# First block of a one-core convolution and two-MLP kernel: all taps of the last 64 channels on TensorE, three tiles slice by slice, zeros while x is loading, and the last sums in halves

## The chip, the cores and the metric

The kernel runs on one core of one Trainium2 chip. The metric is the device time in microseconds of one execution; the time of a kernel is the median of its runs. The engines are called PE (TensorE), DVE (VectorE), ACT (ScalarE), POOL (GpSimd) and SP (SyncE, which here only issues DMAs). "L452" is line 452 of the kernel.

## What is computed

```python
def _attn_ref(x, weight):                 # x (4, 4096, 192), weight (8, 7)
    w = weight - np.max(weight, axis=-1, keepdims=True)
    w = np.exp(w)
    w = w / (np.sum(w, axis=-1, keepdims=True) + 1e-09)
    x_pad = np.concatenate([np.zeros((B, K - 1, D)), x], axis=1)
    idx = np.arange(S)[:, None] + np.arange(K)[None, :]
    x_unf = x_pad[:, idx, :].reshape(B, S, K, H, D // H)
    return np.einsum('hk,bskhg->bshg', w, x_unf).reshape(B, S, D)

def _moe_ref(x, w_gate, w_val, w_out):    # (16384, 192) -> 1536 -> 192
    gate = 1.0 / (1.0 + np.exp(-(x @ w_gate)))
    return gate * (x @ w_val) @ w_out

def _moe2_ref(x, w_in, w_out):            # 192 -> 2048 -> 192
    r = np.maximum(x @ w_in, 0.0)
    return (r * r) @ w_out

# reference: _moe2_ref(_moe_ref(_attn_ref(x, weight)))
```

A causal convolution of seven taps, whose weights are the softmax over a row for each of eight heads of 24 channels, is followed by a gated MLP and by a squared-relu MLP. All is in fp32.

## The kernel before

**Tiling.** The 4096 positions are cut into 32 blocks of 128. A block holds 128 positions of all four sequences, so each matmul streams 512 columns. Activations lie with channels on the partitions. Each fp32 factor is split into a rounded high part and a low part, and a product takes three fast matmuls: high by high, low by high, high by low. The 192 channels are three slices of 64. Slices 0 and 1 ("main") are 128 channels. Slice 2 is called "rest". Two matmuls on 64 rows each, one on the lower and one on the upper half of the partitions, run side by side: L452 and L453 make the gate and the value tile of the first MLP, L499 and L500 (main outputs) and L507 and L508 (rest outputs) sum the outward product in `acc`. I call such two matmuls a pair. A tile of the first MLP takes 9 pairs inward and 5 pairs outward.

**Order of the work.** PE's program is written out by hand. `gated(0)` is the first MLP of block 0: 12 tiles t. After the inward matmuls of tile t come the outward ones of tile t - 3. Tile t may overwrite its PSUM banks when DVE has taken tile t - 2 out of them (`prod_done`). ACT takes the sigmoid of a tile (L693), DVE multiplies it with the value (L851), ACT rounds it (`hi`), DVE subtracts (`lo`, L865). Then `gated(1)`, and a loop over the other blocks in which the second MLP of one block alternates with the first MLP of a later one.

**The first block.** SP loads x of block 0 (rest, then main), then the first weight pieces into four staging buffers. PE makes the softmax weights into per-channel columns `taps` (L621), transposes x (L565 rest, L569 main), and ACT copies the transposed x into `xT` (L705). DVE runs all seven taps of rest (L905, 256 columns each) and four taps of main (L914, L905, 512 columns); PE runs three taps of main as fp32 matmuls with diagonal matrices (L578), which DVE adds (L921). ACT rounds (`x0_hi`), DVE subtracts (L878 main, L882 rest; `x0_lo`). SP then spreads the rest rows to both halves (L309, four DMAs) and swaps the main halves (L300, L301). PE takes the first two tiles slice by slice: slice 0, then slice 2 when spread, then slice 1 when swapped (`first_tiles`).

**The weights.** Weights arrive in pieces; ACT rounds a piece (`piece_hi`, L645), DVE subtracts (`piece_lo`, L839; `first_lo`, L872, for parts of the first three pieces). A piece n from 4 on goes into the buffer of piece n - 4; SP issues piece 4 when all six parts of pieces 0 to 2 have been split (`w1_lo` at 6). In `gated(0)`, `FIRST_AT` sets where pieces 4 to 8 are split: piece 4 stands in ACT's and in DVE's queue ahead of tile 1, piece 5 ahead of tile 2, piece 6 ahead of tile 3. DVE's queue at tile t of `gated(0)` holds, in this order, two taps of the convolution of block 1, the piece, the product of tile t, the subtraction of tile t - 1.

**The end.** After the last sums, ACT copies half of them from PSUM, DVE adds, PE transposes, ACT and DVE copy, and SP stores rest (L334) and then main (L337).

## Time and profile before

| | |
|---|---|
| median of 3 runs | 2346.86 us (2346.43 to 2347.02) |
| the profiled execution's own time | 2346.62 us |
| its span in the trace | 2344.9 us |
| busy share of PE, DVE, ACT, POOL | 99%, 80%, 54%, 6% |
| granted TensorE clock, mean | 1.0 |
| first pair of the stream (L452) starts | 15.75 us |
| last store is issued | 2342.19 us |

The times in the rows below are microseconds from the start of the span, and the span is one execution on the one core. The profiled execution's own time is 1.7 us more than its span, and 0.24 us below the median of the runs. A row of a timeline gives start, duration, engine, line, operation, output and inputs, count, and in brackets how long the engine was idle before it and what released it.

### The profile page before, as it was taken

How to read it: one execution, taken by the hardware profiler on the slowest of the kernel's cores; microseconds unless marked ns; L12 is line 12 of the kernel's file. 1: busy time of each engine (PE TensorE's matmuls, PEld its weight loads, DVE VectorE, ACT ScalarE, POOL GpSimd, SP SyncE). 2: the span in 40 equal slices, each digit the busy share in tenths (PEclk: the TensorE clock that was granted, in tenths of full speed). 3: DMA queues.
4: the chain of work that ended last, by engine and by line, in shares of the span. 5: the costliest groups of instructions: out<-in, count | busy, mean ns of one | idle time of the engine just before them, and what ended most of it. 6: DMA issues, size and time to landing. Idle time of an engine off the chain costs nothing.

```text
span 2344.9 us, 54295 instructions
## 1 busy us (share of the span) xinstructions
PE 2331.7 (99%) x20518; PEld 1923.5 (82%) x20518; DVE 1884.5 (80%) x3969; ACT 1276.0 (54%) x2344; POOL 149.6 (6%) x121
## 2 busy tenths in 40 slices
PE   8999999999999999999999999999999999999999
PEld 6888888888888888888888888888888888888887
DVE  7778778788788787887878878788787787887856
ACT  5545555455554455545555545555555554455556
POOL 2200000000000000000000000000000000000000
PEclk9999999999999999999999999999999999999999
DMA  6111111111110111101111111111111111111101
GB/s 170 42 28 46 30 47 42 31 47 29 49 47 25 47 29 49 47 25 47 36 42 47 33 41 40 36 47 42 31 47 29 47 47 26 47 29 49 41 19 37
DMA packets 93695, 99.28 MB, mean 42 GB/s; under 512 B 8736, under 2 KB 77856, under 8 KB 93664
## 3 DMA queue, kind: packets, MB, share of 16 engines
q1 hardware_dynamic: 93408, 98.27, 16.9%
q10 hardware_dynamic: 256, 0.59, 0.1%
q8 instruction: 20, 0.33, 0.1%
q14 instruction: 11, 0.09, 0.0%
HBM read 19.27 MB, written 12.58 MB: 14 GB/s over the span
## 4 chain that ended last, share of the span: by engine, by line
PE 99%; DVE 0%; DMA 0%; ACT 0%; issue 0%; ACTq 0%; SPq 0%
PE hp L452 55%; PE acc L499 26%; PE acc L507 17%; PE hp L453 1%; PE acc L500 0%; PE acc L508 0%; PE hp L578 0%; DMA xs<-xs 0%; ACT L802 0%; PE hp L621 0%; PE acc L569 0%; DVE xs L878 0%; DVE hid_t L851 0%; DVE z L958 0%; DVE y L921 0%
## 5 line engine op out<-in xcount | busy, mean ns | idle before, releaser
L452 PE MATMUL hp<-xs,w 64*128 64x512 f32 x5760 | 1397.8, 386 | 3.3 <-DVE xs L878 1.5
L453 PE MATMUL hp<-xs,w 64*128 64x512 f32 x5760 | 1397.8, 386 | 0.0
L452 PEld LDWEIGHTS hp<-xs,w 64*128 64x128 f32 x5760 | 1059.6, 184 | 231.0 <-DVE xs L878 1.7
L453 PEld LDWEIGHTS hp<-xs,w 64*128 64x128 f32 x5760 | 1059.6, 184 | 0.0
L865 DVE TENSOR_TENSOR lo<-hid_t,hi 128x512 fp32r<-128x512 f32 x896 | 613.1, 687 | 63.7 <-ACT hi L663 59.5
L693 ACT ACTIVATE act_t<-hp 128x512 f32<-128x512 f32 x384 | 230.1, 599 | 694.9 <-PE hp L452 694.9
L499 PE MATMUL acc<-hi,wo 64*128 64x512 f32 x1792 | 549.0, 386 | 0.0
L500 PE MATMUL acc<-hi,wo 64*128 64x512 f32 x1792 | 549.0, 386 | 0.0
L696 ACT ACTIVATE act_t<-hp 128x512 f32<-128x512 f32 x512 | 302.7, 598 | 186.2 <-PE hp L453 186.2
L851 DVE TENSOR_TENSOR hid_t<-hp,act_t 128x512 f32<-128x512 f32 x384 | 264.9, 690 | 157.3 <-ACT act_t L693 148.9
L499 PEld LDWEIGHTS acc<-hi,wo 64*128 64x128 f32 x1792 | 329.7, 184 | 70.5
L663 ACT CAST hi<-hid_t 128x512 fp32r<-128x512 f32 x512 | 309.7, 611 | 73.2 <-DVE hid_t L855 73.2
L507 PE MATMUL acc<-lo,wo 64*128 64x512 f32 x896 | 345.9, 386 | 0.0
L499 PE MATMUL acc<-lo,wo 64*128 64x512 f32 x896 | 345.9, 386 | 0.0
L508 PE MATMUL acc<-lo,wo 64*128 64x512 f32 x896 | 345.9, 386 | 0.0
L500 PE MATMUL acc<-lo,wo 64*128 64x512 f32 x896 | 345.9, 386 | 0.0
L507 PE MATMUL acc<-hi,wo 64*128 64x512 f32 x896 | 345.9, 386 | 0.0
L508 PE MATMUL acc<-hi,wo 64*128 64x512 f32 x896 | 345.9, 386 | 0.0
L500 PEld LDWEIGHTS acc<-hi,wo 64*128 64x128 f32 x1792 | 329.7, 184 | 0.0
L855 DVE TENSOR_TENSOR hid_t<-act_t 128x512 f32<-128x512 f32 x256 | 176.2, 688 | 144.9 <-ACT act_t L696 142.9
L895 DVE STREAM_TRANSPOSE xT<-xin 32x128 f32<-32x128 f32 x960 | 258.6, 269 | 29.1
L905 DVE SCALAR_TENSOR_TENSOR y<-xT,taps,y 128x256 f32<-128x256 f32 (+1 forms) x381 | 247.7, 688 | 0.3
(83 smaller groups left out, 2141.2 us busy)
## 6 DMA issues: line engine op xcount, KB each, us to landing
xs<-xs SPq DMA_DIRECT2D x160, 256.0 KB, 3.7
xs<-y_rest SPq DMA_DIRECT2D x128, 128.0 KB, 3.0
out_dram<-stage SPq DMA_DIRECT2D x31, 384.0 KB, 2.6
xin<-in_x_dram SPq DMA_DIRECT2D x30, 384.0 KB, 3.4
moved<-y_parts SPq DMA_DIRECT2D x32, 128.0 KB, 2.2
moved<-z_parts SPq DMA_DIRECT2D x31, 128.0 KB, 2.2
stage<-in_moe_w_out_dram SPq DMA_DIRECT2D x7, 384.0 KB, 4.5
stage<-in_moe_w_in_dram SPq DMA_DIRECT2D x12, 128.0 KB, 3.0
```

What stands on the lines that cost most here:

```text
L452: low = pe.matmul(hp[:, 2 * pair, :], w[lower, wk, c], xs[lower, xk, :], start=s, stop=e)
L453: up = pe.matmul(hp[:, 2 * pair + 1, :], w[upper, wk, c], xs[upper, xk, :], start=s, stop=e)
L499: pe.matmul(acc[:, 0, :], w[lower], v[lower], start=s, stop=e)
L500: mm = pe.matmul(acc[:, 2, :], w[upper], v[upper], start=s, stop=e)
L507: pe.matmul(acc[:, 1, :], rest_w[lower], v[lower], start=s, stop=e)
L508: mm = pe.matmul(acc[:, 3, :], rest_w[upper], v[upper], start=s, stop=e)
L663: act.copy(hi[:, t % RING, :], hid_t[:, t % 4, :]).then_inc(hi2_done, 1)
L696: act.activation(act_t[:, t % 2, :], hp[:, 2 * (t // 2 % 2) + t % 2, :], ACT.Relu) \
L851: dve.tensor_tensor(hid_t[:, t % 4, :], hp[:, 2 * (t % 2) + 1, :], act_t[:, t % 2, :], ALU.mult).then_inc(prod_done, 1)
L865: dve.tensor_tensor(lo[:, t % RING, :], hid_t[:, t % 4, :], hi[:, t % RING, :].bitcast(F32), ALU.subtract).then_inc(done, 1)
L895: dve.transpose(dst, src).then_inc(xT_ready, 1)
L905: dve.scalar_tensor_tensor(out=y, in0=src, scalar=w, in1=y, op0=ALU.mult, op1=ALU.add) \
```

## The change

- SP loads x of block 1 into a buffer of its own (`acc_up`) right behind the first weights, instead of waiting until x of block 0 has been transposed. Each part of x has its own semaphore.
- DVE first writes 512 columns of zeros. PE multiplies them five times before it transposes the rest of x, and once behind it (`IDLE`). The two softmax matmuls (L621 before) now stand behind the rest transposes and ahead of the main ones.
- PE takes all seven taps of the rest channels (256 columns, fp32), DVE all seven of the main channels; the addition of the two (L921) is gone. ACT makes seven diagonals for the rest, in place of three for main. ACT and DVE round the rest sums straight from PSUM.
- Three tiles instead of two are taken slice by slice; tile 1 uses two banks of `acc`. The first weight pieces are cut at 384 columns instead of 256 for it. The swap of main is four DMAs of half the size: the high parts can go before the low parts are made. PE's wait for the low parts stands before the third pair of slice 1.
- In SP's queue x of block 2 is loaded behind the swap instead of ahead of it.
- At the end, the copies, additions, transposes and stores of the main channels go in two halves.

The core of the diff:

```diff
-    PE_TAPS = 3
+    FIRST_TILES = 3
+    IDLE = (5, 1)
...
-        pieces = [inward1(k, 0, CHUNK, (2 * P,)) for k in FIRST_SLICES] + [out_piece(w_out1, wo1, 0)]
+        pieces = [inward1(k, 0, CHUNK, (FIRST_TILES * P,)) for k in FIRST_SLICES] + [out_piece(w_out1, wo1, 0)]
...
+        def gate_of(j, t):
+            if isinstance(j, int) and j == 0 and t < 2:
+                return acc[:, 0:2, :] if t else hp[:, 2:4, :]
+            return hp[:, 2 * (t % 2):2 * (t % 2) + 2, :]
...
+            def swap_first():
+                xs = x0_home(0).bitcast(F32)
+                sp.wait_ge(x0_hi, 2)
+                sp.dma_start(xs[lower, 2, :], xs[upper, 0, :]).then_inc(high_swapped, 16)
+                sp.dma_start(xs[upper, 2, :], xs[lower, 0, :]).then_inc(high_swapped, 16)
+                sp.wait_ge(x0_lo, 2)
+                sp.dma_start(xs[lower, 3, :], xs[upper, 1, :]).then_inc(x0_swapped, 16)
+                sp.dma_start(xs[upper, 3, :], xs[lower, 1, :]).then_inc(x0_swapped, 16)
...
             load_x(0)
-            for n in range(FIRST):
+            for n in range(FIRST - 1):
                 load_piece(n)
             load_x(1)
+            load_piece(FIRST - 1)
             spread_x0(0)
+            swap_first()
             load_x(2)
-            swap_x0(0)
...
+                        if part == 2 and xk % 2:
+                            pe.wait_ge(x0_swapped, 32)
...
-                for k in range(PE_TAPS):
+                for k in range(K):
                     pe.wait_ge(tap_square, k + 1)
-                    mm = pe.matmul(hp[:, 2, :].rearrange("p (b s) -> p b s", b=B), diagonals[:, k, :], xT[:, 0:B, k:k + P],
-                                   start=k == 0, stop=k == PE_TAPS - 1)
+                    mm = pe.matmul(rest_conv, diagonals[:, k, :], xT[:, B:G, k:k + P], start=k == 0, stop=k == K - 1)
...
+            pe.wait_ge(zeroed, 1)
+            idle(IDLE[0])
             pe.wait_ge(heads, 8)
+            turn_rest(0)
+            idle(IDLE[1])
             pe.wait_ge(soft, 8)
...
-            turn_x(0)
+            turn_main(0)
             first_taps()
-            turn_x(1)
+            turn_rest(1)
+            turn_main(1)
...
+                elif prev is None and t == 3:
+                    pe.wait_ge(prod_done, 1)
...
             def first_conv():
-                dve.wait_ge(xT_copied, 1)
-                for k in range(K):
-                    tap(0, 1, k, k)
                 dve.wait_ge(xT_copied, 2)
...
+                dve.tensor_scalar(main, xT[:, 0:B, 0:P], taps[:, 0, 0:1], None, ALU.mult).then_inc(conv_step, K + 1)
+                for k in range(1, K):
+                    if k == K - 2:
+                        first_lo(0, 0)
+                    if k == K - 1:
+                        dve.wait_ge(x0_hi, 1)
+                        dve.tensor_tensor(y0_rest[:, 1, :, :], rest_conv, y0_rest[:, 0, :, :].bitcast(F32), ALU.subtract) \
+                           .then_inc(x0_lo, 1)
+                    tap(0, 0, k, K + k)
                 x0_low(0, 2)
+                first_lo(1, 0)
...
+                for half in range(2):
+                    b = slice(half * (B // 2), (half + 1) * (B // 2))
+                    sp.wait_ge(turn_copied, half + 2)
+                    sp.wait_ge(o_last, half + 2)
+                    sp.dma_start(to[:, b, 0:P], o_sb[:, b, 0:P]).then_inc(o_room, 16)
```

In DVE's program the convolution of block 0 stands right behind the copy of `taps`. Before (`y<-xT,taps` is a tap, `w<-stage,w` a part of a weight piece, `xs<-y,xs` the low part of main):

```order
L902 TENSOR_SCALAR y<-xT,taps 128x256 [waits xT_copied,soft]
L905 SCALAR_TENSOR_TENSOR y<-xT,taps,y 128x256 [waits conv_step] x6
L914 TENSOR_SCALAR y<-xT,taps 128x512 [waits xT_copied]
L882 TENSOR_TENSOR y_rest<-y,y_rest 128x256 [waits x0_hi]
L905 SCALAR_TENSOR_TENSOR y<-xT,taps,y 128x512 [waits conv_step] x3
L921 TENSOR_TENSOR y<-y,hp 128x512 [waits conv_step,conv_part]
L872 TENSOR_TENSOR w<-stage,w 128x256 [waits w_hi] x2
L878 TENSOR_TENSOR xs<-y,xs 128x512 [waits x0_hi]
```

The same place of the changed kernel:

```order
L992 TENSOR_SCALAR y<-xT,taps 128x512 [waits xT_copied,soft]
L986 SCALAR_TENSOR_TENSOR y<-xT,taps,y 128x512 [waits conv_step] x4
L953 TENSOR_TENSOR w<-stage,w 128x384 [waits w_hi]
L986 SCALAR_TENSOR_TENSOR y<-xT,taps,y 128x512 [waits conv_step]
L998 TENSOR_TENSOR y_rest<-hp,y_rest 128x256 [waits x0_hi]
L986 SCALAR_TENSOR_TENSOR y<-xT,taps,y 128x512 [waits conv_step]
L959 TENSOR_TENSOR xs<-y,xs 128x512 [waits x0_hi]
```

Seven taps of 256 columns and the addition are gone, three taps of 512 columns are new, and the low part of the rest now stands ahead of the last tap and reads PSUM.

In SP's queue, the DMAs behind the first weights, before (`xs<-y_rest` spreads the rest, `xs<-xs` swaps main, `xin` is x of block 2, the first `stage` load is piece 4):

```order
L309 DMA xs<-y_rest 64x4x128 [waits x0_lo]
L309 DMA xs<-y_rest 64x4x128 x3
L289 DMA xin<-in_x_dram 128x4x192 [waits x_turned]
L300 DMA xs<-xs 64x1024 [waits x0_lo]
L301 DMA xs<-xs 64x1024
L295 DMA stage<-in_moe_w_gate_dram 64x768 [waits w1_lo]
L295 DMA stage<-in_moe_w_val_dram 64x768
```

and in the changed kernel:

```order
L343 DMA xs<-y_rest 64x4x128 [waits x0_lo]
L343 DMA xs<-y_rest 64x4x128 x3
L331 DMA xs<-xs 64x512 [waits x0_hi]
L332 DMA xs<-xs 64x512
L334 DMA xs<-xs 64x512 [waits x0_lo]
L335 DMA xs<-xs 64x512
L313 DMA xin<-in_x_dram 128x4x192 [waits x_turned]
L319 DMA stage<-in_moe_w_gate_dram 64x768 [waits w1_lo]
L319 DMA stage<-in_moe_w_val_dram 64x768
```

The load of x of block 2 (384 KB) has moved from ahead of the swap to right ahead of piece 4, and the swap is four issues instead of two.

## Rows read from the trace of the kernel before

**Rows 1.** The page, busy time of each engine.
```profile
PE 2331.7 (99%) x20518; PEld 1923.5 (82%) x20518; DVE 1884.5 (80%) x3969; ACT 1276.0 (54%) x2344; POOL 149.6 (6%) x121
```

**Rows 2.** The page, costliest group: busy, mean ns, idle before it and its releaser.
```profile
L452 PE MATMUL hp<-xs,w 64*128 64x512 f32 x5760 | 1397.8, 386 | 3.3 <-DVE xs L878 1.5
```

**Rows 3.** Timeline of PE: first inward pair of tiles 4, 5 and 7.
```profile
27.68 0.39 PE L452 MATMUL hp<-xs,w 64*128 64x512 f32 x1
...
30.85 0.39 PE L452 MATMUL hp<-xs,w 64*128 64x512 f32 x1
...
37.20 0.39 PE L452 MATMUL hp<-xs,w 64*128 64x512 f32 x1
```

**Rows 4.** Timeline of DVE: piece 4, then products of tiles 2, 3, 5.
```profile
22.74 0.96 DVE L839 TENSOR_TENSOR w<-stage,w 128x768 fp32r<-128x768 f32 x1 [0.59 <-ACT w L645]
...
26.35 0.68 DVE L851 TENSOR_TENSOR hid_t<-hp,act_t 128x512 f32<-128x512 f32 x1
...
29.48 0.68 DVE L851 TENSOR_TENSOR hid_t<-hp,act_t 128x512 f32<-128x512 f32 x1
...
34.93 0.68 DVE L851 TENSOR_TENSOR hid_t<-hp,act_t 128x512 f32<-128x512 f32 x1
```

**Rows 5.** Windows: stretch, length, DVE busy (instructions), granted clock, DMA share, GB/s.
```profile
18.00:19.00 1.00, 0.86 (x2) 1.00 0.67 258
19.00:20.00 1.00, 0.00 (x0) 1.00 0.74 202
...
22.74:46.50 23.76, 23.58 (x40) 1.00 0.42 113
```

**Rows 6.** Timeline of ACT: piece 4.
```profile
21.88 0.83 ACT L645 CAST w<-stage 128x768 fp32r<-128x768 f32 x1 [0.45 <-DMA stage<-in_moe_w_val_dram]
```

**Rows 7.** Issues of piece 4's second half and of x (block 2), and times to landing.
```profile
18.49 0.60 SPq L295 DMA_DIRECT2D stage<-in_moe_w_val_dram  x1
...
stage<-in_moe_w_val_dram SPq DMA_DIRECT2D x1, 192.0 KB, 3.4
...
xin<-in_x_dram SPq DMA_DIRECT2D x1, 384.0 KB, 3.6
```

**Rows 8.** Timeline of DVE, first block: three main taps; four parts of pieces.
```profile
11.03 2.32 DVE L905 SCALAR_TENSOR_TENSOR y<-xT,taps,y 128x512 f32<-128x512 f32 x3
...
15.71 2.22 DVE L872 TENSOR_TENSOR w<-stage,w 128x256 fp32r<-128x256 f32 x4
```

**Rows 9.** The chain that ended last, first block: start, us.
```profile
13.63 0.69 DVE y L921
...
15.01 0.70 DVE xs L878
```

**Rows 10.** Timeline of ACT, first block: main copy; three diagonals.
```profile
7.11 0.58 ACT L705 COPY xT<-acc 128x512 f32<-128x512 f32 x1 [0.48 <-PE acc L569]
7.59 0.98 ACT L810 ACTIVATE hid_t<-ident,taps 128x128 f32<-128x128 f32 x3
```

**Rows 11.** Timeline of PE: main transposes of blocks 0 and 1; fp32 taps.
```profile
6.01 1.06 PE L569 MATMUL acc<-ident,xin 128*128 128x128 f32 x4
8.14 5.46 PE L578 MATMUL hp<-xT,hid_t 128*128 128x512 f32 x6 [1.07 <-ACT hid_t L810]
...
13.67 0.60 PE L569 MATMUL acc<-ident,xin 128*128 128x128 f32 x4
```

**Rows 12.** Timeline of SP: the four spreading DMAs.
```profile
11.14 2.67 SPq L309 DMA_DIRECT2D xs<-y_rest  x4
```

**Rows 13.** The end: the two last stores, and their times to landing.
```profile
2341.40 0.38 SPq L334 DMA_DIRECT2D out_dram<-stage  x1
2342.19 0.37 SPq L337 DMA_DIRECT2D out_dram<-stage  x1
...
out_dram<-stage SPq DMA_DIRECT2D x1, 256.0 KB, 2.3
out_dram<-stage SPq DMA_DIRECT2D x1, 128.0 KB, 2.0
```

More of the change, by code:

```diff
@@ L444, in _, with into @@
         def _(pe):
-            def into(pair, w, xs, c, order=(0, 1, 2), part=None):
+            def into(banks, w, xs, c, order=(0, 1, 2), part=None):
                 for n, k in enumerate(order):
@@ L451, in into @@
                         s, e = n == 0 and wk == xk, n == 2 and xk % 2 == 1
[L452 to L453 removed]
+                        if part == 2 and xk % 2:
+                            pe.wait_ge(x0_swapped, 32)
+                        low = pe.matmul(banks[:, 0, :], w[lower, wk, c], xs[lower, xk, :], start=s, stop=e)
+                        up = pe.matmul(banks[:, 1, :], w[upper, wk, c], xs[upper, xk, :], start=s, stop=e)
                 return low, up
@@ L460, in first_tiles @@
                     if part:
-                        pe.wait_ge(*((x0_swapped, 32) if FIRST_SLICES[part] == 1 else (x0_spread, 64)))
+                        pe.wait_ge(*((high_swapped, 32) if FIRST_SLICES[part] == 1 else (x0_spread, 64)))
                     pe.wait_ge(w1_lo, part + 1)
-                    for t in range(2):
-                        low, up = into(t, w1, x0_home(0), columns(t), FIRST_SLICES, part)
+                    for t in range(FIRST_TILES):
+                        low, up = into(gate_of(0, t), w1, x0_home(0), columns(t), FIRST_SLICES, part)
                         if part == 2:
@@ L645, in piece_hi, with first_hi @@
                     act.copy(h, staged(n, a, b)).then_inc(w_hi, 1)
+            def first_hi(n, part):
+                act.wait_ge(stage_loaded[n % STAGES], loaded[n])
+                a, b, h, _ = pieces[n][2][part]
+                act.copy(h, staged(n, a, b)).then_inc(w_hi, 1)
             def slot_free(kind, j, t, prev):
@@ L743, in z_copy @@
                     act.wait_ge(out2_done, T2 * NB)
-                    act.copy(acc_up[:, 0, :], acc[:, 2, :]).then_inc(z_copied, 1)
+                    for half in HALVES:
+                        act.copy(acc_up[:, 0, half], acc[:, 2, half]).then_inc(z_copied, 1)
                 else:
@@ L753, in turn_copy_last @@
                 act.copy(o_sb[:, :, P:D], turned_half(0)).then_inc(turn_copied, 1)
-                act.wait_ge(turned, 2)
-                act.copy(o_sb[:, :, 0:R], turned_half(2)).then_inc(turn_copied, 1)
+                for half in range(2):
+                    act.wait_ge(turned, half + 2)
+                    act.copy(o_sb[:, half * (B // 2):(half + 1) * (B // 2), 0:R], turned_main(half)[0]) \
+                       .then_inc(turn_copied, 1)
             def last_of(prev):
@@ L949, in z_add @@
             def z_add(j):
-                last = isinstance(j, int) and j == NB - 1
                 if not (isinstance(j, int) and j == 0):
                     dve.wait_ge(o_turned, O_SQUARES * j)
-                for n in (1, 0) if last else (0, 1):
-                    dve.wait_ge(z_copied, 2 * j + 1 + (1 - n if last else n))
+                for n in range(2):
+                    dve.wait_ge(z_copied, 2 * j + 1 + n)
                     if n:
@@ L1044, in squared @@
                         rest_lo(2, j, t - 1)
+            dve.memset(zeros.bitcast(F32), 0.0).then_inc(zeroed, 1)
             dve.memset(xT[:, :, 0:HALO], 0.0).then_inc(halo_ready, 1)
```

169 lines of the change are left out of this document (96 added, 73 removed).

## The prediction

> **What bounds the kernel now.** I read the page first. PE is busy for 99% of the span [rows 1], and its largest group was idle for 3.3 us in all, 1.5 of them ahead of the very first pair [rows 2]. Nothing between block 0 and the end waits, so the time is the start of PE's stream, plus its waits in block 0, plus the work, plus what follows the last sum. The change touches only the first and the last of these.
>
> Next I took PE's timeline of block 0. One tile of 14 pairs takes 3.17 us (30.85 less 27.68) [rows 3], so a pair takes 0.227. The stream starts at 15.75 and has 41 pairs ahead of tile 4, which are 9.3 us; without a wait tile 4 would start at 25.05. It starts at 27.68 [rows 3]: 2.6 us are lost in waits for the product of a tile and for swapped rows.
>
> Then DVE's timeline, for what PE waits on. Tile 4 needs the product of tile 2, which ends at 26.35 + 0.68 = 27.03 [rows 4], only 0.65 ahead of tile 4. Tile 5 needs that of tile 3, 30.16, which is 0.69 ahead of 30.85 [rows 3, 4]. For tile 7 the lead is 1.6 (35.61 against 37.20). And DVE is not resting: from 22.74 to 46.50 it is busy for 23.58 of 23.76 us [rows 5]. So in block 0 PE cannot run more than 0.65 ahead of now unless DVE's whole row of work moves ahead too. That row starts at 22.74 with the low part of piece 4, behind 0.59 of waiting for ACT [rows 4], which itself waited for piece 4 to land at 21.88 [rows 6]. **The reader is to see here that a load, not the convolution, holds what comes after tile 2.**
>
> **The change, part by part.** All sums go against the profiled execution, whose own time is 2346.62; the median of the runs is 0.24 more.
>
> *Start of the stream.* The main transposes no longer have two rest transposes ahead of them: four take 1.06 [rows 11], so two are about 0.5. ACT's copy of main moves from 7.11 to 6.6 and ends at 7.2 [rows 10]. DVE's seven main taps: three take 2.32 [rows 8], of which 0.7 is the last one's own length, so they follow each other every 0.8, each waiting for the one before. The first is a plain multiply, 0.5 (estimate). 7.2 + 0.5 + 6 x 0.8 = 12.5. A weight part of 384 columns and the low part of the rest stand between taps; four parts take 2.22 [rows 8], 0.55 each, and about half of each hides in the tap's own wait: 0.6 for the two. The convolution ends at 13.1, where now it ends at 13.63 + 0.69 = 14.32 [rows 9]. Rounding main, its low part and PE's start follow as now: L878 starts 0.69 behind the convolution and PE 0.74 behind that. PE starts at 14.5 instead of 15.75.
>
> This holds if the rest sums from PE are there in time. DVE's last tap is queued behind the rest's low part, which waits for ACT's rounding, which waits for PE's seventh tap. Six fp32 records of 512 columns take 5.46 [rows 11], about 0.87 each; 14 of 256 columns would be 6.0 at that pace. But that is the lower of the clock's two levels, 1.2 GHz: the four transposes at 6.01 take 1.06, the same four at 13.67 take 0.60 [rows 11], at 2.4 GHz. (The granted clock reads 1.00 throughout, so only the pace shows it.) ACT's diagonals, 0.33 each [rows 10], are ready by 9.1; at the upper level the last tap then ends near 10, far ahead of 11.5, where it begins to hold DVE. The trace shows PE's dense work from 8.14 becoming fast some 5 us later. [...] I take the upper level; at the lower one the price is 1.4 (below).
>
> *Three tiles by slices.* Slice 0: 9 pairs, 14.5 to 16.6. The rest's low part is made at about 12.3, four spreading DMAs take 2.67 to issue [rows 12] and 2.0 to land if they are like a 128 KB store [rows 13], so slice 2 starts at 16.6 to 16.9 and ends by 19.0. The four swaps are issued until 17.4 and land by 19.5, when PE comes to the first pair that needs low parts. Slice 1 ends at 21.1. Tile 3 needs the product of tile 0 (two steps of 0.6 and 0.7 behind its last pair at 19.5), runs from 21.3 and ends at 23.4. In the kernel before it ends at 27.68 - 5 x 0.227 = 26.55. **PE is 3.1 us ahead here.**
>
> *What is late next.* Outward tile 0 needs the product of tile 1, and ACT and DVE both have piece 4 queued ahead of that. When does piece 4 land? SP issues it when six parts of the first pieces are split: now 15.71 + 2.22 = 17.93 [rows 8]. In the changed kernel L878's successor starts at 13.8, but two parts stand ahead of the copy of the halo, ACT's two copies of block 1's x wait for that halo, and the last three parts wait for ACT behind these copies: 13.8 + 0.6 + 0.9 + 0.8 + 3 x 0.4 + 0.7 = 18.0, and the tolerance of such a sum is 0.3. So 0.1 later, in spite of the earlier convolution. And x of block 2, 384 KB, now goes out at about 17.4, right ahead of piece 4. Alone it took 3.6 to land [rows 7], against 2.0 for 128 KB [rows 13]. Its price for piece 4 lies between 0 (its bytes fit in the gaps: the DMA share is 0.67 and 0.74 from 18 to 20 [rows 5]) and 3.6 - 2.0 = 1.6. I take 0.6, since about half of it fits in these gaps and it has a start of 0.7. Piece 4 lands at 21.9 + 0.7 = 22.6, DVE's row of work starts 0.86 later [rows 4, 6] at 23.5, the product of tile 2 ends 4.3 later, at 27.8, and tile 4 starts then: 0.1 later than now, 0.2 with the slow first pair behind a wait (estimate). Of 3.1 us nothing is left. Bounds: -0.65 - 0.3 = -0.9 and 1.6 + 0.4 - 0.65 = +1.3.
>
> The Trainium skill, "DMA: Bandwidth & Descriptors", section "Queues, rings and completion order", says that each DMA engine consumes a queue's descriptors in ring order, so that a transfer issued ahead is served ahead. By it all of x would pass before piece 4; that is the second rival below.
>
> *The issues of piece 4 and of x* (SP) are hidden otherwise: x of block 2 is read in block 1 only. Zeros write a bank that is overwritten later, and their DVE memset, about 0.5, ends ahead of the first softmax step, which waits for its load. The earlier load of x of block 1 changes places with a weight piece of the same 384 KB, which is needed only near 18.
>
> *The end.* Now the stores go out at 2341.40 and 2342.19, the latter lands in 2.3, and 128 KB take 2.0 [rows 13]. Three stores cost three issues of 0.4: 2341.4, 2341.8, 2342.2. The halves of main are ready by then, since each step is shortened by a third or more. The last is 128 KB: 0.3 gained. Bounds 0 and 0.5.
>
> Sum: 2346.62 + 0.2 - 0.3 = 2346.5 for an execution like the profiled one, 2346.8 as a median.
>
> **The rivals.**
> (1) The clock stays at its lower level through PE's taps. For it: between the zeros and the taps stand only transposes and two tiny products. Then twelve records from 7.5 at 0.43 end at 12.7, rounding and low part move the last tap from 12.3 to 13.7, and all behind it, piece 4 too, by 1.4. Tile 4 starts 1.6 later than now: 2348.1, slower. It decides if the upper level comes later than about 10.
> (2) x of block 2 costs piece 4 its whole transfer, 1.6: tile 4 starts 1.1 to 1.2 later, 2347.8.
> (3) It costs nothing, and the parts are split as early as now: tile 4 at 27.0, 0.65 less and 0.3 at the end, 2345.9.
> (4) DVE's row of work does not bind, as when piece 4 can be taken up earlier or DVE catches up: the 3.1 stay, and 0.3: 2343.5. Against it: DVE has no gap from 22.74 on, and nothing of the change is taken out of that row.
>
> **How the numbers follow.** The likeliest case (2346.3 to 2347.3) has 0.47; rival (1) 0.15, (2) 0.16, (3) 0.15, (4) 0.07. The time is that of the first, 2346.8. The range 2345.4 to 2348.5 takes in (1) to (3) and leaves out (4) and some 0.08 of the rest. No change smaller than 0.2%, 4.7 us, can be told from none; even (4) stays within it. Faster 0.02, slower 0.01, no change 0.97.
>
> **What would show it.** PE's first pair at 14.5; end of tile 3 near 23.4; then a wait of more than 2 us for DVE ahead of the first outward pair and a second ahead of tile 4, which starts at 27.8; piece 4's rounding at 22.6; DVE without a gap behind it; the last store at 2342.1 less or plus what the head gives. Wrong if tile 4 starts before 27.0 or after 28.5, if PE's fp32 records of 256 columns go on at 0.43 behind 10, or if any wait turns up behind block 0.

## The result, and the profile after

| | before | changed |
|---|---|---|
| median, us | 2346.61 (22 runs) | 2349.64 (22 runs) |
| lowest to highest | 2346.43 to 2347.09 | 2347.90 to 2351.76 |
| profiled execution: own time, span | 2346.62, 2344.9 | 2349.22, 2347.5 |
| first pair, tile 4, tile 5, tile 7 start | 15.75, 27.68, 30.85, 37.20 | 13.96, 28.88, 33.70, 40.05 |

The ratio is 1.0014, 95% interval 1.0008 to 1.002. The changed kernel is 3.0 us slower. That is below the 0.2% that the prediction set as its bound, so its "no change" came true, but the time is outside its range of 2345.4 to 2348.5. It also scatters over 3.9 us, where the kernel before scatters over 0.7. Of the twelve runs of variant e17 below, two took 3452 and 9387 us and are left out of its row.

The page of the changed kernel first, busy time and costliest group (rows 1 and 2 of before answer to them):

```profile
PE 2335.6 (99%) x20532; PEld 2130.2 (91%) x20532; DVE 1886.8 (80%) x3967; ACT 1276.6 (54%) x2350; POOL 149.7 (6%) x121
...
L491 PE MATMUL hp<-xs,w 64*128 64x512 f32 x5751 | 1398.7, 387 | 2.6 <-DVE xs L959 2.0
```

This page hides the loss: PE is as busy as before, and its largest group waits less (2.6 us against 3.3 in [rows 2]). PE's waits from 13 to 60 us say more (who waited for whom, us, times, longest):

```profile
PE acc L540 <- DVE lo L946: 2.5, 1, 2.5
PE hp L491 <- DVE xs L959: 2.0, 1, 2.0
PE hp L491 <- DVE hid_t L932: 0.6, 1, 0.6
```

The first and the third, 3.1 us together, lie behind the first pair. That is about what the prediction expected. PE's timeline puts them in place: the taps on PE, the first pair, the last pair of tile 3 and the first outward pair, then tile 4:

```profile
6.28 3.57 PE L636 MATMUL hp<-xT,hid_t 128*128 128x256 f32 x14 [0.27 <-ACT hid_t L775]
...
13.96 0.49 PE L491 MATMUL hp<-xs,w 64*128 64x512 f32 x1 [1.96 <-DVE xs L959]
...
23.99 0.39 PE L491 MATMUL hp<-xs,w 64*128 64x512 f32 x1
...
26.85 0.46 PE L540 MATMUL acc<-hi,wo 64*128 64x512 f32 x1 [2.47 <-DVE lo L946]
...
28.88 0.79 PE L491 MATMUL hp<-xs,w 64*128 64x512 f32 x1 [0.61 <-DVE hid_t L932]
29.48 0.62 PE L491 MATMUL hp<-xs,w 64*128 64x512 f32 x1
29.90 0.62 PE L491 MATMUL hp<-xs,w 64*128 64x512 f32 x1
...
33.72 0.39 PE L491 MATMUL hp<-xs,w 64*128 64x512 f32 x1
...
40.06 0.39 PE L491 MATMUL hp<-xs,w 64*128 64x512 f32 x1
```

The head start is there. Tile 3's last pair starts at 23.99; in the kernel before tile 3 ended at 26.55. But tile 4 starts 1.2 us later than in [rows 3], and behind it pairs follow each other every 0.43 us instead of 0.227. From tile 4 to tile 5 it takes 33.70 - 28.88 = 4.82 us instead of 3.17. From tile 5 on the distance to the kernel before is a constant 2.85.

DVE and ACT, the rows that answer to [rows 4] and [rows 6], show why tile 4 is late (piece 4, then the products of tiles 2 and 3; piece 4 on ACT):

```profile
24.54 0.96 DVE L920 TENSOR_TENSOR w<-stage,w 128x768 fp32r<-128x768 f32 x1 [2.56 <-ACT w L707]
...
28.15 0.68 DVE L932 TENSOR_TENSOR hid_t<-hp,act_t 128x512 f32<-128x512 f32 x1
...
31.27 0.68 DVE L932 TENSOR_TENSOR hid_t<-hp,act_t 128x512 f32<-128x512 f32 x1
```

```profile
23.67 0.84 ACT L707 CAST w<-stage 128x768 fp32r<-128x768 f32 x1 [2.41 <-DMA stage<-in_moe_w_val_dram]
```

Both engines stand for 2.4 and 2.6 us before piece 4, with the products of tiles 1 and 2 queued behind it. SP's timeline, and how long x and the value half of piece 4 took to land, answer to [rows 7]:

```profile
17.21 0.59 SPq L313 DMA_DIRECT2D xin<-in_x_dram  x1
17.84 0.56 SPq L319 DMA_DIRECT2D stage<-in_moe_w_gate_dram  x1
18.45 0.60 SPq L319 DMA_DIRECT2D stage<-in_moe_w_val_dram  x1
...
xin<-in_x_dram SPq DMA_DIRECT2D x1, 384.0 KB, 4.3
...
stage<-in_moe_w_val_dram SPq DMA_DIRECT2D x1, 192.0 KB, 5.2
```

The value half is issued at the time of before (18.45, then 18.49) and takes 5.2 us instead of 3.4. That is the 1.8 by which piece 4 is late.

Windows of one microsecond show the second loss (length, PE busy, PEld, DVE, ACT, POOL, granted clock, DMA share, GB/s):

```profile
14.00:15.00 1.00, 1.00 (x10) 0.83 (x12) 0.93 (x3) 0.03 (x1) 0.00 (x0) 1.00 0.87 201
15.00:16.00 1.00, 1.00 (x8) 0.81 (x6) 0.00 (x0) 1.00 (x3) 0.00 (x0) 0.54 0.88 200
...
18.00:19.00 1.00, 1.00 (x10) 0.83 (x8) 0.70 (x2) 0.00 (x0) 0.00 (x0) 0.75 0.76 161
...
28.00:29.00 1.00, 0.39 (x6) 0.12 (x2) 1.00 (x3) 0.61 (x2) 0.00 (x0) 0.87 0.14 45
29.00:30.00 1.00, 1.00 (x6) 0.81 (x8) 1.00 (x2) 1.00 (x3) 0.00 (x0) 0.50 0.20 74
30.00:31.00 1.00, 1.00 (x8) 0.81 (x6) 1.00 (x3) 0.31 (x1) 0.00 (x0) 0.50 0.54 189
31.00:32.00 1.00, 1.00 (x6) 0.76 (x6) 1.00 (x3) 0.00 (x0) 0.00 (x0) 0.50 0.00 0
32.00:33.00 1.00, 1.00 (x10) 0.81 (x8) 1.00 (x2) 0.18 (x1) 0.00 (x0) 0.92 0.24 55
```

The granted clock is halved, 1.2 GHz, twice: from 15.1 to 18.5, behind the wait ahead of the first pair, and from 28.7 to 32.1, behind 3.1 us of waits. In a busy column both stretches look full; only the clock and the number of matmuls (6 to 8 instead of 10 to 12) show them. The first costs nothing here, since it only shortens the wait for piece 4. The second costs 1.65. Such stretches seem common in the changed kernel: the mean granted clock of this execution is 0.998, and 15 of the 22 runs have the same mean, the other seven 0.999.

**Ledger of the profiled execution:** tile 4 +1.2, the lower clock level behind it +1.65, the end about -0.25: +2.6 in the span. The end's rows answer to [rows 13]:

```profile
2344.16 0.38 SPq L368 DMA_DIRECT2D out_dram<-stage  x1
2344.65 0.97 SPq L373 DMA_DIRECT2D out_dram<-stage  x2
...
out_dram<-stage SPq DMA_DIRECT2D x3, 128.0 KB, 2.0
```

### The profile page after: what moved, and what is told of

Read it like the earlier page. It is cut to its first block, busy times and chain, and to the rows that moved or that the text cites. A ratio compares the mean times of both kernels' runs of the same rounds, so it can differ in the third digit from the quotient of the medians.

```text
span 2347.5 us, 54330 instructions
## 1 busy us (share of the span) xinstructions
PE 2335.6 (99%) x20532; PEld 2130.2 (91%) x20532; DVE 1886.8 (80%) x3967; ACT 1276.6 (54%) x2350; POOL 149.7 (6%) x121
## 4 chain that ended last, share of the span: by engine, by line
PE 99%; DVE 1%; DMA 0%; ACT 0%; issue 0%; DVEq 0%; SPq 0%; ACTq 0%
PE hp L492 50%; PE acc L541 23%; PE acc L549 16%; PE hp L491 6%; PE acc L540 3%; PE acc L548 2%; DMA stage<-in_moe_w_val_dram 0%; DVE y L986 0%; PE hp L611 0%; DVE w L953 0%; ACT xT L771 0%; DVE hid_t L932 0%; ACT w L707 0%; DVE y L983 0%; DVE w L920 0%
## 5 line engine op out<-in xcount | busy, mean ns | idle before, releaser
L986 DVE SCALAR_TENSOR_TENSOR y<-xT,taps,y 128x512 f32<-128x512 f32 x378 | 249.2, 697 | 0.1
```

The costliest lines, as they stand in the source:

```text
L986: dve.scalar_tensor_tensor(out=y, in0=src, scalar=w, in1=y, op0=ALU.mult, op1=ALU.add) \
```

## The experiments

Each ran beside the kernel before, whose median was 2346.86 beside e1, e3, e4 and e5, 2346.63 beside e2, e7, e8 and e9, 2346.78 beside e10, e12, e13 and e14, and 2346.64 beside e15, e16 and e17. These agree within 0.25. The changed kernel itself did not run again beside its variants, so they are compared with its 2349.64 of above. With 11 runs a kernel, the interval of a ratio is about 0.0009 to either side (2.1 us), so small differences are read from the timelines. Variants marked "before" are made from the kernel before, all others from the changed kernel. The starts and the span are those of the one profiled execution of each.

| kernel | median (lowest to highest) | first pair | tile 4 | tile 5 | tile 7 | span |
|---|---|---|---|---|---|---|
| e1 | 2346.78 (2345.92 to 2348.04) | 14.84 | 27.80 | 31.12 | 37.47 | 2345.1 |
| e5 (before) | 2347.91 (2347.59 to 2348.31) | 15.58 | 28.68 | 31.86 | 38.20 | 2345.9 |
| e7 | 2346.78 (2345.88 to 2348.59) | 15.19 | 28.29 | 33.05 | 39.40 | 2346.9 |
| e9 | 2346.51 (2345.42 to 2348.38) | 14.84 | 27.67 | 30.98 | 37.40 | 2344.9 |
| e3 | 2349.32 (2347.20 to 2351.92) | 15.00 | 30.10 | 33.41 | 39.81 | 2347.8 |
| e2 | 2349.93 (2348.59 to 2351.11) | 14.84 | 30.41 | 33.90 | 40.25 | 2347.7 |
| e10 | 2349.12 (2348.90 to 2349.68) | 15.35 | 30.79 | 34.12 | 40.51 | 2347.9 |
| e8 | 2348.19 (2346.21 to 2349.21) | 15.16 | 28.58 | 31.90 | 38.31 | 2347.5 |
| e4 (before) | 2346.48 (2346.27 to 2347.06) | 15.57 | 27.85 | 31.02 | 37.37 | 2344.8 |
| e14 | 2349.76 (2348.87 to 2350.54) | 13.96 | 25.90 | 32.02 | 40.07 | 2347.5 |
| e12 | 2347.84 (2346.53 to 2348.29) | 14.03 | 26.38 | 31.33 | 37.81 | 2345.2 |
| e13 (before) | 2348.28 (2347.85 to 2348.55) | 15.57 | 27.56 | 31.88 | 38.36 | 2346.0 |
| e15 | 2346.65 (2345.90 to 2347.51) | 14.83 | 27.09 | 30.40 | 36.80 | 2345.3 |
| e16 (before) | 2346.62 (2346.32 to 2347.32) | 15.58 | 27.41 | 30.59 | 36.93 | 2344.6 |
| e17 | 2346.05 (2345.07 to 2347.02) | 14.83 | 26.43 | 29.74 | 36.14 | 2345.3 |

### Where x of block 2 is loaded: e1, e5, e7

e1 takes the changed kernel and loads x of block 2 behind piece 6:

```diff
+            for n in range(FIRST, SECOND_HALF + 1):
+                load_piece(n)
             load_x(2)
-            for n in range(FIRST, PIECES1 + 6):
+            for n in range(SECOND_HALF + 1, PIECES1 + 6):
                 load_piece(n)
```

> The changed kernel with one move in SP's queue: x of block 2 is loaded behind pieces 4 to 6 instead of ahead of piece 4. Theory A (the load ahead of piece 4 holds DVE's row of work, and PE's wait for it then costs the clock): piece 4 is rounded at about 22.0 instead of 23.67, tile 4 starts near 27.2 instead of 28.88, the wait ahead of the first outward pair falls from 2.5 to under 1 us, no stretch at half clock behind it, and the time is about 3.2 us less than the changed kernel's 2349.6, so 2346.4. Theory B (the half clock comes from something else, the zeros or the early start): tile 4 starts 1.7 earlier, but the half-clock stretch behind it stays, 2348.0. Theory C (piece 4 is late for another reason, since its own issue is no earlier): no change, 2349.6.

It gives back the whole loss: 2346.78. The value half lands in 3.4 us again, and piece 4 is taken up at 22.58, 1.1 earlier, though this execution's first pair was 0.9 later:

```profile
22.58 0.83 ACT L709 CAST w<-stage 128x768 fp32r<-128x768 f32 x1 [1.62 <-DMA stage<-in_moe_w_val_dram]
```

e5 is the counterpart, the kernel before with its load of x of block 2 moved behind the swap and so right ahead of piece 4:

```diff
-            load_x(2)
             swap_x0(0)
+            load_x(2)
```

> The kernel before with x of block 2 loaded behind the swap instead of ahead of it, as the change does. Theory A (this move alone delays piece 4): piece 4 is rounded 1 to 1.8 us later than 21.88, tile 4 starts 0.4 to 1.2 later than 27.68, and if PE's wait gets long enough the clock falls too: 2347.0 to 2347.8 without the fall of the clock, up to 2349.4 with it. Rival (the delay comes from the four swaps or from the other traffic of the changed kernel): 2346.6.

This one move costs 1.05 us, and none of its runs is as fast as the slowest of the kernel before beside it (2347.34). Piece 4 is taken up at 22.90 instead of 21.88 [rows 6], and tile 4 starts at 28.68, 1.0 later. The clock does not fall in its profile, and the scatter stayed at 0.7.

```profile
22.90 0.83 ACT L645 CAST w<-stage 128x768 fp32r<-128x768 f32 x1 [1.33 <-DMA stage<-in_moe_w_val_dram]
```

e7 loads x of block 2 ahead of the spread instead:

```diff
             load_piece(FIRST - 1)
+            load_x(2)
             spread_x0(0)
             swap_first()
-            load_x(2)
```

> The changed kernel with x of block 2 loaded ahead of the spread of the rest (it is issued near 7 us, when its buffer is free) instead of behind the swap. Theory A (only its place ahead of piece 4 matters): piece 4 is rounded about 3.6 behind its issue as in the kernel before, near 22.2, tile 4 starts at 27.2 to 27.8, and the time is that of the version with the load behind piece 6, 2346.8 or a little less, 2346.3. Rival (any early place collides with the first weights and with x of block 1 and delays the taps): the first pair starts later than 14.8 and the time is 2347.5 or more.

The median is that of e1, 2346.78. Its profiled execution is one of the slowest, 2348.59, and has the lower clock level from 28.0 to 31.4 (tile 4 to tile 5 takes 4.76 us); the fastest runs, 2345.9, are 2.7 below it. So the order of the loads explains the median and not the scatter. The landing of the value half tells the two orders apart in eleven profiles: 5.2 to 5.6 us where x goes out right ahead of it (changed, e2, e3, e14, e15), 3.3 or 3.4 where it does not (before, e1, e7, e9, e12, e17).

### The clock: e3, e2, e10, e8

e3 puts ten matmuls into a bank that is overwritten later, into PE's wait ahead of the first outward pair:

```diff
                     pe.wait_ge(xT_copied, 4)
+                    for _ in range(10):
+                        pe.matmul(acc[:, 3, :], w1[:, 0, 0:P], w1[:, 0, 0:N], start=True, stop=True)
                     pe.wait_ge(prod_done, 2)
```

> The changed kernel with ten matmuls on weights that are already there, written to a bank that is overwritten later, in PE's wait ahead of the first outward pair of block 0 (the output is the same). Theory A (half clock because PE stood still for 2.5 us): the stretch at 0.50 granted clock from 28.9 to 32.1 is gone, tile 4 still starts at 28.9, and 1.5 us are saved: 2348.1, with less scatter. Rival (the clock falls whatever PE does there, or because of what lies before): no gain, 2349.6, or worse by up to 0.5 if the fill delays the outward pair.

The lower level behind the wait is gone in the profile (1.00 from 26 to 32), but the time is the same, 2349.32. This execution was slow in another place: PE's taps took 5.35 us instead of 3.57, and the chain behind them was later by 1.0 at the first pair (15.00) and by 1.2 at piece 4 (taken up at 24.89):

```profile
4.82 1.02 PE L684 MATMUL hp<-soft_w,act_t 8*128 8x7 f32 x4
5.77 1.11 PE L629 MATMUL acc<-ident,xin 128*128 128x128 f32 x4
6.69 5.35 PE L638 MATMUL hp<-xT,hid_t 128*128 128x256 f32 x14
```

These are the paces of the lower level (four main transposes 1.11, against 0.60 at 13.67 in [rows 11]), in spite of the zeros. So both of the prediction's cases happen with the same program up to that place. Among the ten profiles with zeros, PE has the faster pace by 4.8 in three (changed, e12, e14), and only near 11 in seven (e1, e3, e7, e8, e9, e15, e17). Why is not known. No run settles whether it changes from one execution to the next or goes with the chip: e12 and e14 ran on one chip, the seven late ones on three others, and the chip of the changed kernel is not on record. Note that e3's profile loses as much as that of the changed kernel (own times 2349.57 and 2349.22) with no stretch at the lower level behind tile 4: a late start ahead of the late piece 4 costs as much as an early start with the fall behind it.

e2 leaves out the zeros:

```diff
-    IDLE = (5, 1)
+    IDLE = (0, 0)
```

> The changed kernel without the six zero matmuls. Theory A (the zeros decide only when PE's clock first rises, and a fast start is paid back in the wait for piece 4): the softmax matmuls and the fp32 taps run at the slower pace in every run, the first pair starts at 15.0 instead of 13.96, piece 4 and tile 4 move with it by about 1.1, but PE is busier just before and the half-clock stretch behind tile 4 is gone or rarer: 2349.3 to 2350.0, and less scatter than 2347.9 to 2351.8. Rival B (the zeros themselves bring the later fall of the clock, and nothing else is lost): 2348.0. Rival C (the zeros give what they seem to give, 1 us or more of an earlier start): 2350.7 or more.

The median is 2349.93, not to be told from 2349.64. PE's taps take 5.45 us, and the clock falls before the end of the wait of 4.1 us ahead of the first outward pair. So theory A had the time right, but the stretch at the lower level is not gone. Where the clock rises early, the first pair starts at 13.96 instead of 14.84, 0.9 sooner; in seven of the ten profiles with zeros it does not rise early.

e10 is e2 with three fp32 matmuls in the wait ahead of the first outward pair:

```diff
                     pe.wait_ge(xT_copied, 4)
+                    for _ in range(3):
+                        pe.matmul(acc[:, 3, :], ident[:], w1[:, 0, 0:N].bitcast(F32), start=True, stop=True)
                     pe.wait_ge(prod_done, 2)
```

> The changed kernel with its six zero matmuls taken away and three fp32 matmuls on loaded data put ahead of the first outward pair instead, so that the program is as long as the changed one (ten more matmuls had brought one more load of program code at the very end; the output is the same). To be compared with the version without zeros, 2349.93. Theory A (half clock behind tile 4 comes from PE's wait for piece 4): no stretch at half clock from 28 us on in the profile, and 1 to 1.5 us less than 2349.93, so 2348.5 to 2349. Rival (the half clock has another cause): same as without zeros, 2349.9.

The windows of e2 and then of e10 (26 to 32 us, clock in the column ahead of the DMA share):

```profile
28.00:30.00 2.00, 1.86 (x9) 1.61 (x10) 2.00 (x4) 1.77 (x4) 0.00 (x0) 0.50 0.64 190
30.00:32.00 2.00, 2.00 (x16) 1.65 (x14) 2.00 (x5) 1.45 (x3) 0.00 (x0) 0.76 0.34 121
```

```profile
28.00:30.00 2.00, 1.25 (x10) 0.99 (x10) 2.00 (x5) 2.00 (x5) 0.00 (x0) 1.00 0.69 205
30.00:32.00 2.00, 1.40 (x12) 1.03 (x12) 2.00 (x5) 1.62 (x4) 0.00 (x0) 1.00 0.12 45
```

With the wait filled the level stays up, and the scatter falls from 2.5 to 0.8 us. The mean granted clock says the same of all runs: 0.998 or 0.999 in the eleven of e2, 1.000 in nine of e10's and 0.999 in two. This shows that the fall comes from PE standing idle, and that it makes most of the scatter of e2. The median falls by 0.8 only. In e2's profile the slow pairs are mostly the outward ones of tile 0, in a time in which tile 4 would have waited for DVE's product in any case: from the start of piece 4 on DVE, tile 5 is 8.06 us away in e2 and 7.67 in e10. And the 2349.12 of e10 are still 2.3 above the kernel before, without any fall: that part is the late start with piece 4 behind x.

Idleness does not make the clock fall every time (e1 has waits of 2.3, 1.7 and 0.6 us and 1.00 throughout), and the fall is not the only source of scatter. With the zeros in, the runs of the two other kernels with a filled wait still lie 4.7 (e3) and 3.0 us (e8, below) apart, although ten of e8's eleven have a mean clock of 1.000.

e8 is e7 with eight zeros ahead of the first pair and five fills ahead of the first outward pair:

```diff
+                    for _ in range(5):
+                        pe.matmul(acc[:, 3, :], w1[:, 0, 0:P], w1[:, 0, 0:N], start=True, stop=True)
...
             turn_main(1)
+            idle(8)
             gated(0, None)
```

> As e7_x2_early, with eight zero matmuls more ahead of the first pair and five matmuls on loaded weights ahead of the first outward pair (the output is the same). Theory A (what is left of the scatter is half clock after PE has stood still): no stretch at half clock in the first 40 us, and a time of 2346.0 with less scatter, 0.3 under e7_x2_early. Rival (once piece 4 is on time, the clock's falls are hidden in DVE's row, and the fills can only delay the first pair when the clock is low): same as e7_x2_early or up to 0.5 more.

Tile 5 starts at 31.90, 1.15 earlier than in e7, and yet the time is 2348.19, 1.4 more. The loss is at the other end: the last store has been issued at 2343.87, and the span ends 3.6 us later, where in the changed kernel it is 1.9 (2345.62 to 2347.5). The queue that loads instructions has one transfer more than in all other kernels, and it lies right behind that last store:

```profile
q8 instruction: 21, 0.34, 0.1%
```

The program is longer by thirteen matmuls. That the load is the cause is inferred from its place; no run isolates it. (The expectation of e10 puts such a load down to ten more matmuls. Those were e3's, and e3's profile has 20 transfers and the end of the others.)

### The end alone: e4

The kernel before with only the last sums halved.

```diff
...
-                sp.wait_ge(turn_copied, 2)
-                sp.wait_ge(o_last, 2)
-                sp.dma_start(to[:, :, 0:P], o_sb[:, :, 0:P]).then_inc(o_room, 16)
+                for half in range(2):
+                    b = slice(half * (B // 2), (half + 1) * (B // 2))
+                    sp.wait_ge(turn_copied, half + 2)
+                    sp.wait_ge(o_last, half + 2)
+                    sp.dma_start(to[:, b, 0:P], o_sb[:, b, 0:P]).then_inc(o_room, 16)
...
```

> The kernel before with the halved end alone. Theory A: the last store is 128 KB instead of 256 KB and is issued at the same time, 0.3 us less: 2346.3. Rival: the extra instructions and the third store cost as much as the smaller store gives, 2346.6.

The median is 0.38 below that of the kernel before, which the interval alone does not tell from nothing. The profile agrees: tile 7 starts at 37.37 (0.17 later than in [rows 3]) and the span is 0.1 shorter, so 0.3 are gained, as predicted.

### Splitting the first pieces sooner: e9

On top of e7, the last parts of the first pieces are split ahead of the copy of the halo (the last positions of block 0, which the convolution of block 1 needs), on both engines:

```diff
             first_hi(2, 0)
+            for n in range(3):
+                first_hi(n, 1)
             act.wait_ge(halo_ready, 2)
             for n in range(2):
                 xT_copy(1, n)
-            for n in range(3):
-                first_hi(n, 1)
...
             first_lo(2, 0)
-            keep_halo(0)
             for n in range(3):
                 first_lo(n, 1)
+            keep_halo(0)
```

> As e7_x2_early, and the last three parts of the first pieces are split ahead of the copy of the halo and of the copies of block 1's x on ACT and DVE, so that piece 4 can be issued sooner. Theory A (piece 4's landing sets DVE's row of work and so tile 4): the issue of piece 4 moves from 17.9 to 17.2, where SP's four swaps end, and the time falls by 0.5 to 0.7 against e7_x2_early, to about 2345.8, faster than the kernel before. Rival (something else in DVE's row binds, or block 1's x becomes late): no gain.

Piece 4 is on ACT at 22.04 with no wait. Seven runs lie at 2345.4 to 2346.6 and four at 2348.0 to 2348.4, with nothing between. Two cases of the clock would explain that, but it is not shown: the profile is of a run of the faster group, and the mean granted clock reads 0.999 in all four slow runs and in six of the seven fast ones. The median, 2346.51, tells only how many runs fell in which group.

### The pieces on another engine: e14, e12, e13

What remained was rival (4): is the head start worth its 3 us when piece 4 does not stand ahead of the products? e14 gives the low parts of pieces 4 to 6 to GpSimd and splits each a tile later:

```diff
-        FIRST_AT = {1: [4], 2: [5], 3: [6], 4: [7], 6: [8]}
+        FIRST_AT = {2: [4], 3: [5], 4: [6], 5: [7], 6: [8]}
...
+            for n in range(FIRST, SECOND_HALF + 1):
+                (a, b, h, l), = pieces[n][2]
+                pool.wait_ge(w1_lo, split_upto[n - 1])
+                pool.wait_ge(w_hi, split_upto[n])
+                nc.gpsimd.tensor_tensor(l, staged(n, a, b), h.bitcast(F32), ALU.subtract).then_inc(w1_lo, 1)
...
-                        piece_lo(n)
+                        if n > SECOND_HALF:
+                            dve.wait_ge(w1_lo, split_upto[SECOND_HALF])
+                            piece_lo(n)
```

> The changed kernel with the low parts of pieces 4 to 6 made by GpSimd instead of VectorE, and each of the pieces 4 to 7 rounded by ScalarE one tile later. Theory A (after tile 2 only DVE's row of work behind piece 4 holds PE): the wait of 2.5 us ahead of the first outward pair is gone, tile 4 starts near 25.8 although piece 4 lands as late as before, no half clock behind it, and the time is 2346.6 - 1.9 - 0.3 = 2344.4 or up to 1 us more where the clock rises late. Rival (PE is held by DMA or by the clock itself): more than 2347.

It missed by 5 us. Tile 4 did come to 25.90, three microseconds sooner than in the changed kernel, but tile 5 only at 32.02, behind a wait of 2.6 us for DVE's product. The clock was at its lower level from 32.1 to 35.6, so that tile 5 took 4.88 us instead of 3.17, although the expectation had no such stretch. DVE's and GpSimd's timelines show where the wait comes from:

```profile
27.08 4.29 DVE L991 SCALAR_TENSOR_TENSOR y<-xT,taps,y 128x512 f32<-128x512 f32 x2
...
32.48 1.14 DVE L991 SCALAR_TENSOR_TENSOR y<-xT,taps,y 128x512 f32<-128x512 f32 x2
```

```profile
24.78 6.30 POOL L469 TENSOR_TENSOR w<-stage,w 128x768 fp32r<-128x768 f32 x3 [21.37 <-ACT w L712]
```

The same two taps take 4.29 us beside GpSimd and 1.14 behind it; 4.29 is about the length of two of its instructions (2.1 each). The Trainium skill, "SBUF — State Buffer", section "SBUF: two separate sides", says that the two engines share a pair of ports under an exclusive lock, taken by a DVE instruction with two SBUF inputs against a GpSimd one that reads SBUF. By it each tap waits for a whole GpSimd instruction, and the rows agree.

e12 adds e14's edit to e9, and e13 adds it to the kernel before.

> As e14_after_pool, with x of block 2 loaded ahead of the spread and the last parts of the first pieces split ahead of the halo copy. Theory A: piece 4 is early, and nothing stands between the tiles: tile 4 starts near 25.4, time 2344.0, the fastest so far. Rival (with DVE's row gone, the start and the swaps bind and the earlier piece 4 gives nothing more): the same as e14_after_pool.

> The kernel before with the same move of three low parts to GpSimd. It tells what the change to the first block is worth once DVE's row does not bind. Theory A: the waits ahead of tile 4 in the kernel before (swapped rows, product of tile 0) stay, 25.05 + 2.3 = 27.4 for tile 4, only 0.3 less than now: 2346.3, so that the changed head is worth some 2 us over it. Rival (the kernel before gains as much, and the changed head gives nothing even then): 2344.5.

Both missed for the same reason: PE stands for 1.48 and 0.99 us ahead of tile 5, for DVE's product. e13 costs the kernel before 1.5 us.

### The same order without GpSimd: e15, e16, e17

These change only the line `FIRST_AT` above. The splits stay on ACT and DVE and stand one tile later: e15 on the changed kernel, e16 on the kernel before, e17 on e9.

> The changed kernel with the splits of pieces 4 to 7 (on ScalarE and on VectorE) one tile later in their order, and nothing on GpSimd. VectorE then takes product 1 and its low part in the 2.6 us in which it stood before piece 4 at 22 to 24.5, and the outward product of tile 0 can follow tile 3 at once. Theory (the head start of the new first block is real, 2.3 us, and was lost only because piece 4 stood ahead of product 1): tile 4 at 26.0 instead of 28.88, tile 5 at 29 to 30.5 instead of 33.70, no stretch at the lower clock level behind them, VectorE then sets the pace (0.95 for a piece + 0.6 + 0.6 + 0.95 for the taps, 3.1 a tile); 2345.5 in all, between 2344.3 and 2347. Rival (the head start is used up later whatever stands there: VectorE's whole row of pieces, products and taps until 45 us has no room): tile 4 at 26 but the tiles from 7 on at or behind their place, 2348 to 2349.6.

> The kernel before with the same one edit of the order, nothing on GpSimd. Its tile 3 ends at 26.55 and its tile 4 starts at 27.68, so only 1.1 of wait is there to be won at tile 4, less what VectorE's row binds at tiles 5 to 7 (0.1 to 0.2 each). Theory: tile 4 at 27.3 to 27.7, 2346.4 (2345.8 to 2346.9). It should lie 1 to 2.3 us above the changed kernel with the same edit if the head start is real; the rival has the two the same, or the changed one slower as it was without the edit.

> The same edit on the version with x of block 2 loaded ahead of the spread of x of block 0 and the last splits of the first pieces ahead of the copy of the halo. Piece 4 lands about 1.6 us sooner there, so less hangs on the order: theory 2345.0 (2343.8 to 2346.5), tile 4 at 25.8 to 26.2, the same as the changed kernel with the edit or up to 0.5 faster, and less scatter than the 3 us of the version without the edit if the stretch at the lower clock level comes from the wait at tile 4. Rival (the scatter comes from when the clock first rises): scatter of 2 to 3 us as before.

e15 takes off all of the loss: 2346.65, 3.0 less than the changed kernel, with x of block 2 where it was. DVE now works in the time in which it stood (the product of tile 1, a low part and two taps, then piece 4):

```profile
21.67 0.69 DVE L932 TENSOR_TENSOR hid_t<-acc,act_t 128x512 f32<-128x512 f32 x1
22.35 0.69 DVE L946 TENSOR_TENSOR lo<-hid_t,hi 128x512 fp32r<-128x512 f32 x1
22.97 0.74 DVE L983 TENSOR_SCALAR y<-xT,taps 128x512 f32<-128x512 f32 x2
25.47 0.96 DVE L920 TENSOR_TENSOR w<-stage,w 128x768 fp32r<-128x768 f32 x1 [1.76 <-ACT w L707]
```

The outward product of tile 0 follows tile 3 without a wait. PE still waits 1.9 us ahead of tile 4 for the product of tile 2, which stands behind piece 4, so tile 4 is 1.1 later than expected; the clock does not fall there. The scatter falls to 1.6. e16 leaves the kernel before as it was, 2346.62: it had nothing to gain there. So the theory of e15 was half right. The head start is real and was lost at piece 4, but e15 did not come out below e16. e17 shows the rest, in the profile of the slowest of its ten runs. There tile 4 starts at 26.43 and tile 7 at 36.14, 1.06 ahead of [rows 3], and yet the span is 0.4 longer than before. From tile 7 to the end it takes 2309.2 us, in e15 2308.5, and in the changed kernel 2307.45. PE's waits in e17:

```profile
PE hp L491 <- DVE xs L959: 2.9, 1, 2.9
PE hp L491 <- issue: 0.9, 1, 0.9
PE hp L491 <- DVE hid_t L932: 0.2, 1, 0.2
```

The second and the third stand behind tile 7, and e15 has the same two. One is for DVE's product at 42.88 (43.53 in e15), behind DVE's pairs of taps. This is the rival of e15, and a small part of the time. The other ends at 54.73 in e15 as in e17, though PE comes to it 0.6 us apart, and the profile names no releaser. The record has one all the same. The pair at 54.73 is the first of block 1, and in PE's program it waits for the four DMAs that spread the rest rows of block 1 (`x0_spread`). The last of them is issued at 50.15 in e17 and lands 4.5 us later, at 54.65; in e15 it is issued at 50.82 and lands 3.8 later, at 54.62. In e9 it lands at 54.2, ahead of PE, which starts the pair at 54.41 without a wait; in e16 at 52.3, with PE there at 53.93. So the head start of block 0 runs into the spread of block 1. That this landing ends the wait is read from these times; no run moves the spread.

## Why the prediction was wrong, point by point

- **Start of the stream, 14.5.** The mechanism was right. The start was 13.96 in the profiled execution, where DVE's first main tap began at 6.77 and not at 7.2: the main transposes ahead of it ran at the upper level too (0.66 us for the four). It was 14.8 to 15.2 in seven profiles of variants with zeros, where rival (1)'s clock came true, with 4.62 (e17) to 5.54 us (e7) for PE's taps instead of 3.57. Rival (1)'s price was then 0.9 to 1.2 and not 1.4.
- **"I take the upper level".** This was a choice that held in the profiled execution by luck as much as by the zeros. No run shows that zeros bring the upper level by the time of the taps: it was there in three profiles of ten, and e2 shows that in the median the zeros bring nothing that can be measured.
- **Tile 3 ends at 23.4, 3.1 us ahead.** It ended at 24.2, 2.3 ahead, because of the first stretch at the lower level.
- **"I take 0.6, since about half of it fits in these gaps".** This is the term that was mis-sized. Piece 4 was issued on time, not 0.1 late, but x of block 2 cost it 1.8 us, more even than the upper bound of 1.6. Piece 4 was taken up at 23.67 instead of 22.6, and tile 4 started at 28.88 instead of 27.8. That was rival (2), put at 0.16 and 2347.8; e1 and e5 show it by putting x elsewhere and by adding it to the kernel before (1.0 there, where x goes out 1.9 us ahead of the value half, not 1.24). The Trainium skill, "DMA: Bandwidth & Descriptors", section "Queues, rings and completion order", has descriptors consumed in ring order; 5.2 us against 3.4 agrees with it, and the gaps in an average DMA share do not speak against it.
- **The wait was costed as a wait only.** The prediction had PE stand for more than 2 us ahead of the outward pair and again ahead of tile 4, and took "0.2 with the slow first pair" for it. The clock fell to 1.2 GHz behind it, and the next 3 us ran at half pace: +1.65. No step of the sum had this, nor a rival, and by rival (2) alone the time would have stayed within the range. Together with rival (2) it gives the 2.6 measured in the span. e10 against e2 shows that PE's standing idle brings the fall; e1 and e15 have shorter waits ahead of the first outward pair (1.7 us and none) and no fall. How the 3.0 of the median divide is less sure, since e3's profile loses as much by a late start (rival (1)) together with rival (2) and without a fall behind tile 4. A rival that joined the two was missing as well.
- **DVE's row binds.** This was right: DVE has no gap from 24.54 to 52 us, and tile 4 follows the product of tile 2 by 0.05.
- **The end, -0.3.** This was right (e4: -0.38 in the median, 0.3 in the profile).
- **Rival (4).** The head start could be freed only in part: e15 and e17 win 3.0 and 3.6 over the changed kernel, but from tile 7 on they take 1.0 and 1.7 us longer, most of it for DVE's product and for the spread of block 1's rest rows.

What stays open: what decides whether the clock rises by 4.8 or near 11 us in the same program, what decides whether it falls behind a wait, and which of the two makes how much of the scatter with zeros. The best version tried, e17 at 2346.05, is 0.6 below the kernel before, ratio 0.9996 (0.9987 to 1.0006), and so not told from it.

## What to carry to other kernels

When a stage is sped up, look at the load that is queued first behind it on every engine: here piece 4 stood in ACT's and DVE's order ahead of products that did not need it, and a bulk load of no urgency had been put right ahead of it. A head start turns into a wait, and the waits of 3.1 us on TensorE cost half as much again here through its clock, so price a wait with the slower stretch that can follow it, and ask whether the transfers of the next block are early enough for the head start to last. Before moving work to GpSimd, price what it does to VectorE's instructions with two SBUF inputs beside it. And a scatter that grows from 0.7 to 3.9 us is itself a finding: read more than one profile.

## What the runs showed of the hardware

- Piece 4's value half (192 KB) landed 5.2 us after its issue with 384 KB issued 1.24 us ahead of it in the same queue, and in 3.4 without. Nine further profiles give 5.2 to 5.6 us with it and 3.3 or 3.4 without. In e5, where the 384 KB went out 1.9 us ahead, it took 4.3.
- The granted clock was 0.50 from 28.7 to 32.1 behind waits of 2.5 and 0.6 us, and stayed at 1.00 in e10, where three matmuls lay in the wait. It did not fall behind every such wait: e1 has 2.3, 1.7 and 0.6 us of waits and 1.00 all along.
- Two VectorE taps of 128x512 took 4.29 us beside GpSimd subtractions (e14; 4.33 in e13) and 1.14 without.
- A longer program had one instruction load more at its end and 1.7 us more between its last store and the end of the span (e8 against the changed kernel).
